# Shifting work among VectorE, ScalarE and the load queue at the end of a banded-attention stage

## The reference

```
scores = q k^T / 8 - slope[h] * dist          # dist: row minus column, or n_local
keep   = column < n_global (8)  or  0 <= row - column < n_local (96)
a      = softmax(where(keep, scores, -1e9));  x = a v          # x: 2 x 768 x 512
gate   = sigmoid(causal depthwise conv of x, 5 taps)
y      = ((gate * (x @ w_val)) @ w_out)
h      = relu(y @ w_in);  gate2 = sigmoid(depthwise conv of h, 3 taps)
out    = (h * gate2) @ w2                                       # 2 x 768 x 512
```

## Time and profile before

| | us |
|---|---|
| median of 3 runs | 269.46 |
| lowest and highest | 267.98, 269.72 |
| the profiled execution's own time | 269.72 |
| its span in the profile | 267.9 |
| PE busy in the span | 261.0 |
| DVE, ACT, POOL busy | 190.0, 151.6, 47.4 |

### The profile page before, as it was taken

The page is one execution under the profiler, slowest core; times in us unless marked ns, Lnnn a source line. Parts: engine busy times, 40 slices in busy tenths (PEclk is TensorE's granted clock), DMA queues, the critical chain, the costliest instruction groups (busy, mean ns, idle before and its releaser), DMA issues.

```text
span 267.9 us, 4415 instructions
## 1 busy us (share of the span) xinstructions
PE 261.0 (97%) x1526; PEld 205.9 (77%) x1526; DVE 190.0 (71%) x467; ACT 151.6 (57%) x346; POOL 47.4 (18%) x70
## 2 busy tenths in 40 slices
PE   8899999999999989999999999999999999999995
PEld 7444558788778878888888888888888888888883
DVE  0388479999889977998950897988409998991000
ACT  1051569889998767343554407965537649753100
POOL 1012056695387621200000000000000000000000
PEclk9999999999999999999999999999999999999999
DMA  6999807686897111000000000000000003004021
GB/s 199 355 377 315 289 7 208 203 259 191 240 262 232 45 43 42 4 1 0 2 0 0 0 2 0 1 0 0 2 0 0 0 2 132 24 0 159 0 100 57
DMA packets 20263, 25.16 MB, mean 94 GB/s; under 512 B 3728, under 2 KB 10384, under 8 KB 20112
## 3 DMA queue, kind: packets, MB, share of 16 engines
q1 hardware_dynamic: 19088, 23.86, 27.9%
q10 hardware_dynamic: 1152, 1.01, 1.1%
HBM read 21.52 MB, written 3.34 MB: 93 GB/s over the span
## 4 chain that ended last, share of the span: by engine, by line
PE 85%; DVE 6%; DMA 4%; ACT 3%; issue 1%; ACTq 1%
PE ps L559 21%; PE ps L561 20%; PE ps L560 20%; PE ps L455 8%; PE ps L530 6%; PE ps L515 5%; PE ps L502 5%; DMA win<-in_win 4%; DVE prob L949 2%; ACT prob L699 1%; DVE probT L956 1%; DVE total_eps L960 1%; DVE g L977 1%; DVE xT L972 0%; ACT probT L706 0%
## 5 line engine op out<-in xcount | busy, mean ns | idle before, releaser
L699 ACT ACTIVATE prob<-prob,low 128x256 f32<-128x256 f32 (+1 forms) x96 | 45.9, 482 | 6.6 <-DVE low L949 6.4
L977 DVE SCALAR_TENSOR_TENSOR g<-xT,cw,g 128x512 f32<-128x512 f32 x48 | 34.3, 779 | 1.6 <-ACT g L734 1.6
L805 ACT ACTIVATE h<-ps 128x512 f32<-128x512 f32 x24 | 14.0, 595 | 31.2 <-PE ps L561 31.2
L949 DVE CUSTOM_DVE_ANT_0 prob<-ps,bias 128x256 f32<-128x256 f32 x80 | 30.4, 408 | 1.7 <-PE ps L502 1.7
L455 PE MATMUL ps<-win,w1t 128*128 128x512 f32 x56 | 24.7, 596 | 1.0 <-DMA win<-in_win 1.0
L559 PE MATMUL ps<-gh,Wh 128*128 128x512 f32 x64 | 24.9, 389 | 0.0
L561 PE MATMUL ps<-gh,Wl 128*128 128x512 f32 x64 | 24.9, 389 | 0.0
L561 PE MATMUL ps<-hghA,w2l 128*128 128x512 f32 x64 | 24.9, 389 | 0.0
L560 PE MATMUL ps<-hglA,w2h 128*128 128x512 f32 x64 | 24.9, 389 | 0.0
L559 PE MATMUL ps<-hghA,w2h 128*128 128x512 f32 x64 | 24.9, 389 | 0.0
L560 PE MATMUL ps<-gl,Wh 128*128 128x512 f32 x64 | 24.9, 389 | 0.0
(11 more groups left out here) (101 smaller groups left out, 527.7 us busy)
## 6 DMA issues: line engine op xcount, KB each, us to landing
q_rows<-in_q SPq DMA_DIRECT2D x12, 256.0 KB, 4.8
kW<-in_k SPq DMA_DIRECT2D x12, 256.0 KB, 5.2
v_own<-in_v SPq DMA_DIRECT2D x12, 256.0 KB, 3.3
invT<-inv_turned SPq DMA_DIRECT2D x20, 128.0 KB, 3.4
out<-xT SPq DMA_DIRECT2D x5, 512.0 KB, 2.8
w<-in_w SPq DMA_DIRECT2D x8, 256.0 KB, 11.0
v_win<-in_v SPq DMA_DIRECT2D x10, 192.0 KB, 3.3
prob<-in_wval SPq DMA_DIRECT2D x1, 1024.0 KB, 9.6
```

Source lines behind the costliest of these rows:

```text
L699: act.activation(part, part, ACT.Exp, scale=-1.0, bias=low[:, t % 2, i:i + 1], accum_out=total[:, t % 2, i:i + 1]).then_inc(exp_done, 1)
L805: act.activation(h_cols(m, c), pieces(HB(m), c), ACT.Relu).then_inc(relu_done, 1)
L949: dve.tensor_tensor_reduce(prob[:, t % 2, i, cols], SC(f, e)[:, i % HH // 2, cols], table, -SCALE, 3.0e38, ALU.add, ALU.min, low[:, t % 2, ...
L977: dve.scalar_tensor_tensor(out=pieces(g[:, m, :], c), in0=x_cols(m, c, tap - PAD1), scalar=cw1[:, m, tap:tap + 1], in1=pieces(g[:, m, :], ...
```

## The change

Four edits. The early steps begin in iteration 6 and there are two of them in odd iterations: one, two, one, two, one in iterations 6 to 10, seven in all, and one is left for the end. From tile 5 on, the copy of pair (t, 3) moves from DVE to ACT, between exp(t+1, 2) and exp(t+1, 3); the semaphore counts follow it. On SP, q and k of tile t+4 are loaded before the sums of tile t are waited for, the sums are sent and spread without any load between, and v of tile t+4 (it was t+3) is loaded behind them.

```diff
-EARLY_STEPS = {t: 1 for t in range(TAPS_FROM + 3, TILES - 1)}
+EARLY_STEPS = {t: 1 + t % 2 for t in range(TAPS_FROM + 1, TILES - 1)}
+THIRD_COPY_FROM = TAPS_FROM
...
+        def t0_pairs(t):
+            return (0, 2, 3) if t >= THIRD_COPY_FROM else (0, 2)
+
         def copied(t, j):
-            return (t0_copied, t1_copied)[j % 2], 2 * t + j // 2 + 1
+            if j in t0_pairs(t):
+                return t0_copied, sum(len(t0_pairs(u)) for u in range(t)) + t0_pairs(t).index(j) + 1
+            return t1_copied, sum(PAIRS - len(t0_pairs(u)) for u in range(t)) + j // 2 + 1
...
-            def send_inverse(t):
+            def turn_inverse(t):
                 slot = t % 2
                 sp.wait_ge(inverse_done, t + 1)
                 sp.dma_start(inv_turned[t]..., inv_rows[:, slot, :]).then_inc(inv_sent[slot], 16)
-
-            def spread_inverse(t):
-                slot = t % 2
                 sp.wait_ge(inv_sent[slot], 16 * (t // 2 + 1))
                 if t >= 2:
                     sp.wait_ge(x_ready, t - 1)
...
                 for t in range(TILES):
-                    send_inverse(t)
-                    if t >= 1 and t - 1 + RING < TILES:
-                        load_v(t - 1 + RING)
                     if t + RING < TILES:
                         load_q(t + RING)
                         load_k(t + RING)
-                    spread_inverse(t)
+                    turn_inverse(t)
+                    if t + RING < TILES:
+                        load_v(t + RING)
...
                     exp_of(t + 1, 2)
+                    if 3 in t0_pairs(t):
+                        copy_t0(t, 3)
                     exp_of(t + 1, 3)
...
                 copy_t0(TILES - 1, 2)
+                copy_t0(TILES - 1, 3)
...
                     score(t + 1, 4)
-                    copy_t1(t, 3)
+                    if 3 not in t0_pairs(t):
+                        copy_t1(t, 3)
...
                 copy_t1(TILES - 1, 1)
-                copy_t1(TILES - 1, 3)
```

## The result

The change makes the kernel slower: 277.38 us median against 269.11, a ratio of 1.032 (95% interval 1.027 to 1.037). 269.0 was forecast and the range ended at 270.4. Measured again later, the ratio was 1.019 (1.014 to 1.024). The two intervals do not meet, so the loss varies between 2 and 3%. The profiled execution took 274.83 us with a span of 273.0, so its trace shows 5.1 us of loss, of the 8.3 us between the medians.

A forecast was written before the change was run, and what follows sets the result against it. PE was taken to bound the kernel. Terms of +0.27 (iterations 6 and 7), -0.09 (iteration 9) and -0.91 + 0.29 (iteration 10 and transition) gave -0.44 us, from 269.46 to 269.0 us; range 267.7 to 270.4.

The forecast's parts named there:

- What bounds the kernel: Whole kernel: PE is the bound, busy for 261.0 of the span's 267.9 us.
- the ceiling of 2.0 us for a gain: PE's iterations 6 to 10 with the transition: excess of 1.98 us, so the change saves 2.0 us at most.
- The third copy on ACT, +0.27 us: ACT, full in iteration 6, delays PE at the 76.37 us stop by 0.27 us; bounds zero and 0.5.
- Steps for copies on DVE: DVE, iterations 7 to 9: three steps replace three copies, 16.83 us becomes 16.98; two collisions of 0.7 us taken.
- the stop of iteration 10: PE waits at turn(10, 3) for ACT's copy, DVE being late: 0.29 us forecast instead of 0.57.
- The steps taken from the end: DVE after 102.79 us: worth nothing, since five steps took 3.39 us and DVE still waited 0.68 us for pv(11).
- The SP order: SP's loads: PE gets no wait for q, k or v; 0 us, bounds -0.1 and +0.3, only through collisions.
- the waits that I had named as signs of being wrong: Signs against the forecast: PE waiting for q, k or v; steps of 1.3 us in most of iterations 7 to 9.
- The slower rival: POOL blocks DVE's steps in iterations 7 and 9: 271.1 us with all five blocked, 270.4 with four; chance 0.16.
- The chance of 0.04 for slower by 1%: Whole time: chance 0.04 of slower by more than 1%, as part of the 0.16 for POOL blocking the steps.

The follow-up runs named there:

- The best version found: Kernel before with the third copy on ACT from tile 8 and block 1's first tap moved from iteration 6 to 7: ratio 0.996, again 0.9954.
- the bad case above: The changed kernel itself, profiled and timed once more: profiled execution 280.56 us, median 275.94 against 269.54 us.
- The experiment with four rows: The changed kernel with `inv_rows` four deep instead of two, so `turn_inverse` waits for the send of four tiles before: 274.27 against 269.93 us.
- the first of the versions above: Changed kernel with v between send and wait, third copy from tile 7, one early step in each of iterations 6 to 10: 268.92 against 269.56 us.

## Why the prediction was wrong

- **What bounds the kernel, and the ceiling of 2.0 us for a gain: right as far as tested.** The best version found has 1.2 of it in the stretches, and the dense part kept its length in the changed kernel (167.29 us).
- **The third copy on ACT, +0.27 us: right in size, wrong in place.** I put it at the stop of turn(7, 3), and that one stayed at 0.3 us. PE met it one iteration earlier, in pv(6), which needs the copy itself: iteration 6 took 4.73 or 4.74 us instead of 4.46 in every version that had the copy from tile 5, but for the bad case above. Iteration 7 is another matter: 6.22 us with the steps and 6.42 with the copy alone, against 6.21 before.
- **Steps for copies on DVE, and the stop of iteration 10: right in the sum.** With SP's old order the sum was -0.44 us, which was the forecast, with two terms off by 0.2 us each way; the seven steps alone cost 1.6 us of the timed median, the copy alone gives 0.5 of the stretches. The gain of 0.44 does not show in the medians, so it is right as a reading of one trace, not as a time.
- **The steps taken from the end, worth nothing: right.** After the last copies one step was left and DVE then waited 3.9 us for pv(11), instead of 0.68.
- **The SP order: this is the step that failed.** I wrote that every load is gated only by things done earlier and put the edit at 0, bounds -0.1 and +0.3. I asked of each load whether its condition held in time, and not how long SP needs for one tile when everything in it runs one after the other. SP's timeline of before had the terms: seven issues beside the send, some 3.7 us, of which the 2.4 us of loads between the send and the wait were cover; and a send that took 2.0 us (at 38.04) to 4.2 (at 70.88). With the cover gone the send is added whole, which makes 5.7 to 7.9 us against PE's 5.82. So a loss of up to 2 us a tile was to be seen as possible, though not its size; measured were sends of 3.3 to 4.2 us and turns of 7.2 to 8.0. The term that I put at 0 came to 6.1 us in the profiled executions: iterations 6 to 10 took 34.81 us with the new order and 28.69 with the old one, all else kept. My text also had k of tile 10 issued at about 70 us, earlier than before; it was issued at 80.75, against 73.41 before. "The sums are sent and spread without any load between" was in my own description of the change; what it removed was the work that hid a wait.
- **Nor did I ask who waits for SP.** `turn_inverse` on DVE waits for the send of two tiles before, and my text said only that PE doesn't wait for q, k or v. It never did in the changed kernel: none of the waits that I had named as signs of being wrong is the one that came. The experiment with four rows shows that without this wait late k would have cost 4 us all the same.
- **The slower rival** was POOL blocking the steps. Blocked instructions exist (1.18 us for a small sum in the first of the versions above), but none of the loss shows without the SP order: steps and copy with the old order are level (1.001), the order alone has all of it (1.025).
- **The chance of 0.04 for slower by 1%** was the price of bounding an unknown too closely: the edit with the least working had the narrowest bounds.

## What to carry to other kernels

An issue queue is an engine: add up one full turn of it, waits for its own DMAs included, and compare that with the period of the engine that sets the pace. When a send and the wait for it are moved together, whatever stood between them was hiding the transfer. A queue that is too slow by 2 us a turn shows nothing at first, because buffers absorb it; look at what it waits for (the engine that feeds it, or its own transfers), not only at who waits for it.

## What the runs showed of the hardware

- A 16 KB write to DRAM took 2.0 to 2.2 us to be seen by its waiter with no load in flight (100.31 in the changed kernel, 88.07 and 94.33 before), 3.3 to 4.2 us right behind v, q and k (changed kernel), 2.8 to 4.0 behind q and k alone (v between the send and the wait), and up to 4.4 on another queue. The size is the same each time, so it is not what sets the time.
- The granted clock fell to 0.50 after a stop of PE of 1.78 us, when PE was already busy again, and cost a further microsecond in qk (3.02 against 2.00 us) in the kernel with the new SP order alone. After stops of 1.45 to 2.15 us in the profiled execution of the changed kernel it stayed at 1.00, so a stop of this size can do it and need not.
- A VectorE instruction of 8 columns can wait as long for GpSimd as a step of 512: it took 1.18 us against 0.17 alone, the step of the earlier trace rows 1.42 against 0.75. The Trainium skill, SBUF — State Buffer, section Who interferes with whom, names `tensor_scalar` among the instructions that can enter a two-port mode, if their operands allow it, and then contend with GpSimd for the shared port pair; by that rule the trace agrees, though no run shows the mode itself.
